# Scores of single heads in the two row halves of TensorE, with queries loaded once

## What is computed

```python
# for each token t, all heads
m_new = maximum(f_gate + m, i_gate)
f_stab, i_stab = exp(f_gate + m - m_new), exp(i_gate - m_new)
C = f_stab * C + i_stab * outer(v, k)          # state, 40 x 40 per head
n = f_stab * n + i_stab * k
y = sigmoid(o_gate) * (C @ q) / maximum(abs(n @ q), 1)
# then, with x = y of all heads side by side (320 wide), for each token
e = argmax(x @ w_gate), or the expert of the token before where x @ w_local says so
out = p[e] * (relu(x @ w1[e]) @ w2[e])         # 8 experts, hidden 1024
```

## Time and profile before

| | us |
|---|---|
| median of three runs | 253.44 |
| the profiled execution | 252.62 |
| its span (first to last instruction) | 250.3 |
| TensorE busy | 231.1 (92%) |
| TensorE weight loads | 185.4 (74%) |
| VectorE busy | 175.1 (70%) |
| ScalarE busy | 126.6 (51%) |
| GpSimd busy | 73.8 (30%) |

### The profile page before, as it was taken

How to read it: one execution, slowest core, us unless ns; L and a number is a source line. 1 busy time by engine, 2 the same in 40 slices (tenths; PEclk the granted TensorE clock), 3 DMA queues, 4 the chain that set the end, 5 groups by cost and what they waited for, 6 DMA issues and landing times.

```text
span 250.3 us, 5795 instructions
## 1 busy us (share of the span) xinstructions
PE 231.1 (92%) x2216; PEld 185.4 (74%) x2217; DVE 175.1 (70%) x366; ACT 126.6 (51%) x198; POOL 73.8 (30%) x81
## 2 busy tenths in 40 slices
PE   4989999799999999969999899999999799999970
PEld 1677887698988888838987778888888585667640
DVE  5699679999899899975779966986856852120230
ACT  2233756968968669216444144576763524334110
POOL 7074302606107200051001350552334353230111
PEclk9995899999999999999999999999999999999998
DMA  5999629899799674359400449788317110110000
GB/s 142 279 225 350 158 37 333 238 295 376 153 285 327 119 320 148 107 155 415 183 3 12 126 100 382 212 294 326 134 58 222 44 33 12 58 34 4 8 29 23
DMA packets 12918, 42.30 MB, mean 169 GB/s; under 512 B 2259, under 2 KB 4366, under 8 KB 12890
## 3 DMA queue, kind: packets, MB, share of 16 engines
q1 hardware_dynamic: 10890, 37.40, 48.1%
q0 software_dynamic: 1824, 4.35, 5.0%
q10 hardware_dynamic: 176, 0.17, 0.3%
HBM read 38.37 MB, written 4.98 MB: 173 GB/s over the span
## 4 chain that ended last, share of the span: by engine, by line
PE 63%; DMA 13%; DVE 12%; ACT 5%; issue 4%; POOL 0%; POOLq 0%; ACTq 0%; DVEq 0%
PE psU L1179 15%; DMA out<-rows,srcid 8%; PE psO L1000 6%; PE psS L970 6%; PE psS L1154 6%; PE psO L1140 4%; PE psA L868 4%; PE psU L981 3%; PE psS L1140 3%; DMA xt<-x_rows,srcid 2%; PE psM L924 2%; PE psU L864 2%; PE psU L1054 2%; PE psA L961 2%; PE psA L958 2%
## 5 line engine op out<-in xcount | busy, mean ns | idle before, releaser
L1179 PE MATMUL psU<-W,hidT 128*128 128x320 f16 (+1 forms) x384 | 54.9, 299 | 2.4 <-DVE hidT L1732 2.0
L1179 PEld LDWEIGHTS psU<-W,hidT 128*128 128x128 f16 x384 | 37.0, 98 | 17.2 <-DVE hidT L1732 2.4
L584 POOL DMA_INDIRECT out<-rows,srcid x11 | 17.7, 1612 | 53.9 <-ACT rows L791 47.9
L1000 PEld LDWEIGHTS psO<-W,hidT 128*128 128x128 f32 x192 | 25.8, 197 | 1.9 <-issue 0.3
L970 PE MATMUL psS<-W 104*128 104x256 f32 x96 | 24.7, 389 | 0.0
L1000 PE MATMUL psO<-W,hidT 128*128 128x41 f32 x192 | 24.6, 278 | 0.0
L1140 PE MATMUL psO<-xT,W 128*128 128x128 f16 x384 | 22.8, 219 | 0.7 <-DVE xT L1648 0.7
L1140 PEld LDWEIGHTS psO<-xT,W 128*128 128x128 f16 x384 | 21.7, 98 | 1.5 <-DVE xT L1648 1.3
L536 POOL TENSOR_TENSOR W<-W 128x640 f32<-128x640 f32 x5 | 6.7, 1330 | 48.0 <-DMA W<-in_kvo 40.0
L704 ACT ACTIVATE hid<-psA 128x512 f32<-128x512 f32 x24 | 14.3, 595 | 12.4 <-PE psA L963 12.1
L638 ACT ACTIVATE W<-stage 128x1024 f16<-128x1024 f32 (+1 forms) x14 | 16.0, 1146 | 8.1 <-DMA stage<-in_w 8.0
(11 more groups left out here) (254 smaller groups left out, 452.0 us busy)
## 6 DMA issues: line engine op xcount, KB each, us to landing
stage<-in_w SPq DMA_DIRECT2D x11, 640.0 KB, 4.7
W<-in_w SPq DMA_DIRECT2D x10, 512.0 KB, 6.7
W<-in_kvo SPq DMA_DIRECT2D x5, 968.0 KB, 6.6
stage<-in_w SPq DMA_DIRECT2D x9, 512.0 KB, 7.3
W<-in_w SPq DMA_DIRECT2D x4, 640.0 KB
rows<-in_w SPq DMA_DIRECT2D x5, 512.0 KB
W<-in_qk SPq DMA_DIRECT2D x6, 416.0 KB
x_rows<-rows SPq DMA_DIRECT2D x12, 192.0 KB, 5.0
```

The source lines that it names most:

```text
L584: pool.indirect_dma_start(out[:, :], bass.IndirectOffsetOnAxis(ap=rows_of, axis=0), ybuf, None, bounds_check=TOK - 1, oob_is_err=False).th ...
L1000: last = mm(own[j % 2][:, h], prob[j % 2][:, h], vb[u][:, QUAD * j + h], start=True, stop=True)
L1179: last = mm(psU[:, 0:DM], h[:, k * P:(k + 1) * P], w, start=(k == 0 and n == 0), stop=(k == FC - 1 and n == 2))
```

## The change

Heads get other places: heads 0 to 3 take slots 0 to 3 of the upper half, heads 4 to 7 the same slots of the lower half, heads 8 to 11 and 12 to 15 slots 4 to 7. A score call now serves two groups: for each of four slots one matmul of 40 rows in the upper half, into PSUM bank 0, and one in the lower half, into bank 1, with 128 moving columns each. There are two such calls a chunk, at the places of scores 0 and 1 and of scores 2; the place of scores 3 is empty. Queries are loaded once, by one DMA, into a stacked buffer that both the scores and the old part read. The block-diagonal buffers, their clearing and ScalarE's copies are gone. The old part's output is written so that its heads stand in their old order. A buffer `room` keeps the space of the removed ones, so that the others stay where they were.

```diff
@@ -82,7 +82,7 @@
 def place(bh):
 
 
-    return bh // 2, 64 * (bh % 2)
+    return QUAD * (bh // (2 * QUAD)) + bh % QUAD, 64 * (bh // QUAD % 2)
 
 
 def build(nc, gates, qk, kvo, w1, w2, wr, cb, cf, xs, out):
...
@@ -141,10 +141,10 @@
 
             return take(freed, n, dt, parts)
 
-        qpairs = [over(2 * HALF).rearrange("p (a g t) -> p a g t", a=2, g=BH // 2) for _ in range(2)]
-        kraw, qraw = [over(HALF) for _ in range(2)], over(HALF)
+        kraw, qraw = [over(HALF) for _ in range(2)], [over(HALF) for _ in range(2)]
+        room = over(3 * HALF)
         kstack = [v.rearrange("p (g t) -> p g t", g=BH // 2) for v in kraw]
-        qstack = qraw.rearrange("p (g t) -> p g t", g=BH // 2)
+        qstack = [v.rearrange("p (g t) -> p g t", g=BH // 2) for v in qraw]
         kvob = [early(KVO_N), over(KVO_N)]
         slots = [stage[:, 0], stage[:, 1], over(PIECE)]
         vb = [v[:, 0:BH * V].rearrange("p (h d) -> p h d", h=BH) for v in kvob]
...
@@ -426,8 +424,7 @@
 
                 q, k = qk[c, :, 0], qk[c, :, 1]
                 sp.dma_start(kraw[u][0:PAIR], k).then_inc(s_kq[u], 16)
-                sp.dma_start(qpairs[u][0:64, 0].rearrange("p g t -> p (g t)"), q[0:64]).then_inc(s_kq[u], 16)
-                sp.dma_start(qpairs[u][64:PAIR, 1].rearrange("p g t -> p (g t)"), q[64:PAIR]).then_inc(s_kq[u], 16)
+                sp.dma_start(qraw[u][0:PAIR], q).then_inc(s_kq[u], 16)
 
             def load_values(c, u):
 
...
@@ -501,10 +498,6 @@
 
         @block.gpsimd
         def _(pool):
-            for u in range(2):
-                pool.memset(qpairs[u][0:64, 1], 0.0).then_inc(s_qz, 1)
-                pool.memset(qpairs[u][64:PAIR, 0], 0.0).then_inc(s_qz, 1)
-                pool.wait_ge(s_qz, 2 * (u + 1))
             pool.memset(kS, 0.0).then_inc(s_zero, 1)
 
             def split_rows(c):
...
@@ -651,14 +644,6 @@
                 nc.scalar.activation(r[:, DUP:DUP + 64], xw[:, b, 256:DM], ACT.Copy,
                                      scale=inv[:, b:b + 1]).then_inc(s_xr, 1)
 
-            def stack_queries(c):
-
-                u = c % 2
-                act.wait_ge(s_kq[u], 48 * (c // 2 + 1))
-                wait_if(act, s_old, 2 * (c - 1))
-                nc.scalar.copy(qstack[0:64], qpairs[u][0:64, 0]).then_inc(s_qs, 1)
-                nc.scalar.copy(qstack[64:PAIR], qpairs[u][64:PAIR, 1]).then_inc(s_qs, 1)
-
             def late_high(n):
 
                 e, i = late_piece[n]
...
@@ -962,24 +945,25 @@
                            start=False, stop=False)
                     mm(psA[:, j % 2], identb, masknegb, start=False, stop=True).then_inc(s_arg, 1)
 
-                def scores(j):
-
-                    wait_if(pe, s_p, NQ * c + j - 1)
-                    for i in range(QUAD // 2):
-                        g = QUAD // 2 * j + i
-                        last = mm(psS[:, j % 2, 2 * i * P:2 * (i + 1) * P], kstack[u][0:PAIR, g],
-                                  qpairs[u][0:PAIR, :, g], start=True, stop=True)
-                    last.then_inc(s_sc, 1)
+                def scores(m):
+
+                    wait_if(pe, s_p, NQ * c + 2 * m)
+                    for h in range(QUAD):
+                        g = QUAD * m + h
+                        for a in range(2):
+                            r = slice(64 * a, 64 * a + D)
+                            last = mm(psS[:, a, h * P:(h + 1) * P], kstack[u][r, g], qstack[u][r, g], start=True,
+                                      stop=True)
+                    last.then_inc(s_sc, 2)
 
                 def old_part(n):
 
-                    pe.wait_ge(s_qs, 2 * c)
                     pe.wait_ge(s_cbd, 2 * c + 2)
                     wait_if(pe, s_osc, 2 * c + n - 2)
                     for i in range(QUAD):
                         g = QUAD * n + i
-                        last = mm(old[:, 2 * i:2 * i + 2].rearrange("p h d -> p (h d)"), qstack[0:PAIR, g],
-                                  Cbd[0:PAIR, g].rearrange("p a d -> p (a d)"), start=True, stop=True)
+                        last = mm(old.rearrange("p (a h) d -> p h a d", a=2)[:, i], qstack[u][0:PAIR, g],
+                                  Cbd[0:PAIR, g], start=True, stop=True)
                     last.then_inc(s_old, 1)
 
                 def own_part(j):
...
@@ -1003,14 +987,12 @@
                 pe.wait_ge(s_al, c + 1)
                 if c < 2:
                     pe.wait_ge(s_pad, c + 1)
-                    pe.wait_ge(s_qz, 2 * (c + 1))
                 wait_if(pe, s_exp, NQ * c - 1)
                 busy(0, FILL_FIRST)
                 exponents(0)
                 exponents(1)
-                pe.wait_ge(s_kq[u], 48 * (k + 1))
+                pe.wait_ge(s_kq[u], 32 * (k + 1))
                 scores(0)
-                scores(1)
                 if c == 0:
                     factors(0, 1)
                 else:
...
@@ -1025,7 +1007,7 @@
                     own_part(1)
                 if c > 1:
                     x_transposes(2 * (c - 1), 0, c - 1)
-                scores(2)
+                scores(1)
                 if c == 1:
                     x_transposes(0, 0, 0)
                 if c > 0:
...
@@ -1035,7 +1017,6 @@
                 exponents(3)
                 if c > 0:
                     logits(2 * (c - 1))
-                scores(3)
                 if c == 0:
                     factors(1, 2)
                 if c == 1:
...
@@ -1942,7 +1923,8 @@
 
     def by_dim(x):
 
-        return x.reshape(BH // 2, 2, NC, P, D).transpose(2, 1, 4, 0, 3)
+        x = x.reshape(2, 2, QUAD, NC, P, D).transpose(3, 1, 5, 0, 2, 4)
+        return x.reshape(NC, 2, D, BH // 2, P)
 
 
 
...
@@ -1980,8 +1962,8 @@
     parts["reset1"][:] = (np.arange(LAST_E * N1) % N1 > 0)
     parts["jrow"][:] = ((np.arange(DYN)[:, None] + 4 + 2 * np.arange(E)) * P).reshape(-1)
     parts["vrow"][:] = (np.arange(DYN) + 3) * P + BIG
-    parts["maskg"][0:BH] = heads // 2 == np.arange(BH // 2)
-    parts["selp"][0:BH] = heads % 2 == part // 64
+    parts["maskg"][0:BH] = np.array([place(bh)[0] for bh in range(BH)])[:, None] == np.arange(BH // 2)
+    parts["selp"][0:BH] = np.array([place(bh)[1] for bh in range(BH)])[:, None] // 64 == part // 64
     tile = np.arange(NT)
     parts["ids"][:, 0::2] = tile * P - NOID
     parts["ids"][:, 1::2] = part[:, None]
```

More of the change, by code:

```diff
@@ L274, in build @@
         s_cst, s_gates = sem("consts_loaded"), sem("gates_loaded")
-        s_kq = [sem(f"keys_and_query_pairs_loaded_{u}") for u in range(2)]
-        s_qs = sem("queries_stacked")
+        s_kq = [sem(f"keys_and_queries_loaded_{u}") for u in range(2)]
         s_id = sem("small_identity_loaded")
@@ L291, in build @@
         s_zero = sem("key_pad_cleared")
-        s_qz = sem("query_pairs_cleared")
         s_split, s_al = sem("split_step"), sem("split_rows_ready")
@@ L759, in step @@
                         tile_high(0)
-                if c + 1 < NC:
-                    stack_queries(c + 1)
             def first_hidden_high(t):
```

## The result

The changed kernel takes 261.56 us (median of four runs, 258.17 to 266.4), the kernel before beside it 253.04 (251.93 to 255.98). The ratio is 1.032, 95% interval [1.024, 1.039], with the most disturbed runs left out. It is slower; 251.1 was forecast, with a range up to 256.0. The profiled execution took 263.07 us, span 261.0.

The account below looks back on a forecast made before the run. The prediction took the attention chunks as bound by TensorE, with VectorE close behind. Chunks 0 to 5 gave +0.9 - 1.1 + 0.1 - 0.4 - 0.5 - 0.5 = -1.5 us, so 252.6 - 1.5 = 251.1 us, range 247.7 to 256.0.

Parts of the forecast that it names:

- (c): TensorE's clock in chunk 0 or 2: one more 6.8 us stretch at half, up to 3.4 us more; chance 0.14.
- (d): TensorE's clock: the existing half-clock stretch from 19.5 to 26.3 us is gone, up to 3.4 us less; chance 0.13.
- Row halves run together: Score calls: upper-half and lower-half matmuls overlap, 1.10 us a call with mode entry and exit, saving 1.36 us a chunk.
- rival (b): Score calls: row halves run one after the other, 1.96 us a call, +5.2 us in all, about 257.8; chance 0.07.
- The state update: Update outputs go four to one column half, then four to the other, losing pairing: +0.9 us in chunks 0 to 4.
- rival (a): State update keeps its column-half pairs, so its added time goes: 2.6 us less, 248.5 us; chance 0.21.
- The joined scores: Both groups' scores released together: first weighing 0.2 to 0.3 us late at no cost, VectorE's 0.54 us own-part-0 wait gone.
- Chunks 3 and 4: Attention chunks: scores -1.36 and update +0.9 give -0.4 us in chunk 3, -0.5 in chunk 4.
- Chunk 1: VectorE's first score wait stays; its waits of 0.64 and 0.67 us for third and fourth scores go, about -1.1 us.
- chunk 0: First attention chunk: the longer state update lies on the chain into chunk 1, +0.9 us.
- Chunk 5: Last attention chunk, without update: the scores' -1.36 us is cut by VectorE's idle 0.84 to about -0.5.
- ScalarE's copies, memsets, SP's third DMA: Removed query copies, four GpSimd memsets and one DMA a chunk: counted as zero, at most 1 us for the copies.

Follow-up runs that it names:

- the stretches: Two runs of the changed kernel with extra matmuls of several shapes ahead of chunk 0; in one, 480 half-row records took 27.07 us, 240 of 104 rows 26.96.
- doubled pairs: The changed kernel with its half-row score matmuls issued twice in each call: 270.93 us (259.78 to 275.13).
- 128-row fillers: The changed kernel with six more 512-column fillers a chunk, three ahead of exponents 0 and three at the empty place: 261.27 us (255.69 to 267.0).
- the fillers of chunk 1: The changed kernel with five 512-column filler matmuls at the empty place in chunk 1 alone: 272.66 us (251.64 to 277.91).
- the old scores: The kernel before with group 3's scores issued right behind group 2's in chunk 1 alone: 255.73 us, ratio 1.015 [0.996, 1.035].

## Why the prediction was wrong

**The step that failed** is the clock. The sum took it as in the kernel before, and its rivals on it were two. (c) was one more stretch at half like the one from 19.5 to 26.3 us (6.8 us at 0.50, TensorE busy for all of it), in chunk 0 or 2, where VectorE sets the pace: by my estimate up to 3.4 us, half of 6.8, which gives 254.5, and 256 with the longer update; its chance was 0.14. (d) was that stretch gone, up to 3.4 us less, at 0.13. There were 34.1 us at half in chunks 1 and 2, which made these chunks 3.0 and 9.3 us longer, besides 6.8 from the end of attention on, most of it in fillers ahead of a wait. What starts the long fall is shown: the scores of group 3 are gone from between the logits and the factor transposes of chunk 1, and in ten profiles of ten that reach this hole at full clock it falls, in none of four with fillers there. The prediction counted the emptied place as time saved and did not ask what its work did for the clock; chunk 1 was in neither rival.

Why the clock stays down for 34.1 us is in part argued. The change put 2.2 us of half-row pairs a chunk in place of 3.56 us of 104-row scores; in the stretches pairs kept a full clock (27 us) and did not restore a fallen one (42.7 us at half), while 104-row matmuls did, in 4.3 us. The rest of a chunk is fillers, exponents, and load-bound matmuls, of which 104-row ones lost the clock by themselves after 4.9 to 6.3 us. For the chunks it rests on doubled pairs not helping while 128-row fillers do, with wide scatter. No run put 104-row scores back into the changed kernel, and the kernel before without fillers ahead of its own parts stood at half for 23.9 us too.

**Row halves run together**: right, 1.09 us a call (1.73 before), so rival (b) is out. That this equals the forecast 1.10, which has 0.23 us in it for the way in and out of 64-row work, is luck. That there is such a cost the logits of the earlier trace rows show at the change itself:

```profile
59.48 0.57 PE L924 MATMUL psM<-W,xT 128*128 128x9 f32 x3
...
59.67 0.39 PE L924 MATMUL psM<-W,xT 64*128 64x9 f32 x2
59.99 0.39 PE L868 MATMUL psA<-cbf 128*128 128x512 bf16 x1
```

The last 128-row record starts at 59.48 us and the first of 64 rows 0.19 later; the second and last of these starts at 59.80 and the filler behind it 0.19 later, where from one 128-row record to the next it is 0.11. With the 0.10 us ahead of a call and the 0.11 behind, a call costs 1.30. The stretches give the stream alone as 16 x 27.07 / 480 = 0.90, so what comes on top is 0.40 and not 0.23. The scores save 0.96 us a chunk, not 1.36.

**The state update**: direction right, size wrong: +0.31 us, not +0.9. The order of the heads is the cause, since alternating them gives 1.06 us again; by the estimate above four to seven tenths of the pairing survive in runs of four, part of what rival (a) has.

**The joined scores** start the first weighing late, as said: it begins 2.84 us after chunk 3 does, and began 2.60 after. I had this costing nothing, and VectorE's wait for own part 0 gone. It waits 0.48 us for the scores and 0.38 for own part 0, in sum what it waited before (0.86 against 0.87). Its idle time in chunks 3 and 4 is 1.24 and 1.26 us, where under 1 was forecast; TensorE, never idle in chunk 3, still sets the pace.

**Chunks 3 and 4** at full clock: -0.6 and -0.7 us, forecast -0.4 and -0.5. They came out near because two errors cancel. In chunk 3 the scores give -1.38 at the calls and +0.42 beside them, the update +0.31: -0.65, where the prediction had -1.36 + 0.9. **Chunk 1** can be compared up to its fall. From the chunk's first filler to the filler of own part 2 it is 14.00 us before (22.79 to 36.79) and 13.23 after (23.48 to 36.71): 0.8 less of the 1.1 forecast. The row behind the 0.64 us there names an instruction of VectorE's own as its releaser, not the scores, as the prediction has it. Its score call ends at 32.45, just ahead of the weighing at 32.54, so the scores may well be what it waited for, but a wait of 0.39 us is still there; the later one for the fourth group is gone:

```profile
32.83 0.69 DVE L1355 TENSOR_TENSOR hidT<-psS,hid 128x512 f32<-128x512 f32 x1 [0.39 <-DVE W L1331]
...
35.72 0.68 DVE L1355 TENSOR_TENSOR hidT<-psS,hid 128x512 f32<-128x512 f32 x1
```

In **chunk 0** the update crosses the fall at 20.0 us, and the chunk ends 0.7 us later, forecast 0.9; it also begins 0.24 us later (7.78 against 7.54). **Chunk 5** does not give the 0.5 us forecast. Its last logits at half clock take 1.45 us (118.98 to 120.43) and took 0.84, so the chunk is 0.1 us longer even without that: TensorE waits 0.76 us for VectorE's routing, a wait that was not there before:

```profile
116.55 0.29 PE L932 MATMUL psO<-W,rows 128*128 128x8 bf16 x6 [0.76 <-DVE rows L1600]
```

**ScalarE's copies, memsets, SP's third DMA**: nothing of them shows in chunks 3 and 4, but no run isolates them. Open.

**At equal clock** the runs do not settle which kernel is faster. At 0.931 the changed one took 258.2 us, the kernel before 261.2, and 265.5 at 0.933; at 0.937 the changed one took 261.4, the kernel before 260.6 at 0.938. With the fillers of chunk 1, the run at 0.964 was 1.6 to 4.3 us under five of the kernel before. A saving at full clock is shown in chunks 3 and 4 alone.

## What to carry to other kernels

In this kernel dense work of 104 and 128 rows did two jobs: its own, and holding the clock (104-row matmuls held it at full for 27 us by themselves; without the fillers ahead of its own parts the kernel before stood at half for 23.9 us). Before taking such work out of a place, look at what is left around it (here logits, a wait of 0.48 us and 16-row transposes), and price the loss of the clock by a whole stage at half speed (here 9.3 us in one chunk), not by one short stretch. When a part comes out as forecast, redo its terms: here two wrong ones cancelled. A single profile is one draw: take the granted clock of every run, and compare kernels at equal clock and in how often they lose it.

## What was not expected of the hardware

- Matmuls of 40 rows in one half alone, with records that leave no gap, lost the full clock in 3.5 us (from 197.8 to 201.3); two such streams in the two halves held it for 27 us, and left a fallen one at half for 42.7 us. 104-row ones of 128 columns restored it in 4.3 us.
- Matmuls of 104 rows and 41 columns, one weight load each, lost it after 4.9 to 6.3 us in three stretches, though TensorE's records have no gap (46.60 of 46.60 us busy, mean clock 0.55). So a TensorE that is busy without a gap in the profile can lose its clock.
- At the hole in the dense work of chunk 1 the clock falls in ten profiles of ten, one of them with the old scores; how long the fall lasts varies from 3.4 to 37.5 us.
- Column halves in runs of four lose little against strict alternation: 400 update records take 13.1 us (0.033 each), alternating 11.7 (0.029), where records of 104 rows with 128-column loads take 0.112. In the kernel's own update it is 1.37 against 1.06.
- Row halves run two at a time (480 records of 40 rows in 27.07 us, 240 of 104 rows in 26.96), but going in and out costs 0.10 us ahead of a call and 0.11 behind, where it shows as longer work of others.
- The kernel before does not keep a full clock either: over 43 runs its mean clock is 0.931 to 0.996 and its time 249.0 to 265.5 us.
